# Attention in steps of two duos with its multiplications on GpSimd, and another order around the gather, in a one-core attention and expert kernel

## The reference

```python
scores = scale * q @ k.T                      # per batch and head
keep = (key < n_sink) | (0 <= query - key < window)
a = exp(where(keep, scores, -1e9) - max)
a = a / (sum(a) + 1e-9)
x = (a @ v) as 1536 rows of 512
y = ((x @ w_a) * (x @ w_b)) @ w_out
logits = y @ w_gate                           # 8 experts
# greedy by descending logit: each token to one expert, 192 a expert
out[tokens of e] = relu(y[tokens of e] @ w1[e]) @ w2[e]
```

## Time and profile before

| | us |
|---|---|
| median of 3 runs (lowest, highest) | 624.77 (624.16, 624.82) |
| the profiled execution's own time | 624.48 |
| its span in the profile | 622.6 |
| busy PE | 609.3 (98%) |
| busy DVE, ACT, POOL | 438.1, 290.6, 318.4 |
| PE's share of the chain that ended last | 95% |

### The profile page before, as it was taken

How to read it: one execution, slowest core, us unless ns; L and a number is a source line. 1 busy time by engine, 2 the same in 40 slices (tenths; PEclk the granted TensorE clock), 3 DMA queues, 4 the chain that set the end, 5 groups by cost and what they waited for, 6 DMA issues and landing times.

```text
span 622.6 us, 13278 instructions
## 1 busy us (share of the span) xinstructions
PE 609.3 (98%) x4704; PEld 504.7 (81%) x4704; DVE 438.1 (70%) x1428; ACT 290.6 (47%) x692; POOL 318.4 (51%) x230
## 2 busy tenths in 40 slices
PE   8999999999999999999999999999899999999995
PEld 6666668999899899989977887777677888888894
DVE  6888883333246619999898998888946667766670
ACT  6889883333333332332332224243526756567540
POOL 7566563455455546554456551000094876667741
PEclk9999999999999999999999999999989999999998
DMA  8374231333554364454214151413459578876500
GB/s 277 110 290 147 80 95 55 109 109 102 172 168 122 117 206 133 134 189 120 68 36 153 52 187 37 152 52 114 175 202 386 184 221 294 296 242 238 189 26 25
DMA packets 76096, 94.35 MB, mean 152 GB/s; under 512 B 4448, under 2 KB 53888, under 8 KB 75392
## 3 DMA queue, kind: packets, MB, share of 16 engines
q1 hardware_dynamic: 73696, 86.82, 42.5%
q0 software_dynamic: 2048, 6.29, 3.1%
q10 hardware_dynamic: 288, 0.41, 0.2%
HBM read 87.16 MB, written 6.34 MB: 150 GB/s over the span
## 4 chain that ended last, share of the span: by engine, by line
PE 95%; DVE 2%; POOL 1%; issue 1%; ACT 0%; POOLq 0%; DVEq 0%
PE bank L1392 15%; PE bank L1269 14%; PE bank L1271 13%; PE bank L1270 13%; PE bank L1492 8%; PE bank L1515 5%; PE bank L1256 4%; PE bank L1196 4%; PE bank L1216 4%; PE bank L1494 4%; PE bank L1282 2%; PE bank L1434 2%; PE bank L1343 1%; PE bank L1172 1%; PE bank L1261 1%; PE bank L1474 1%
## 5 line engine op out<-in xcount | busy, mean ns | idle before, releaser
L537 POOL TENSOR_TENSOR wl_ab<-raw_ab,wh_ab 128x1024 fp32r<-128x1024 f32 x46 | 110.1, 2393 | 107.7 <-ACT wh_ab L650 107.7
L1269 PE MATMUL bank<-xh,wh_ab 128*128 128x384 f32 x384 | 131.9, 343 | 0.0
L1271 PE MATMUL bank<-xh,wl_ab 128*128 128x384 f32 x384 | 128.7, 335 | 0.0
L1270 PE MATMUL bank<-xl,wh_ab 128*128 128x384 f32 x384 | 128.6, 335 | 0.0
L607 POOL TENSOR_TENSOR w2l<-w_raw,w2h 128x1024 fp32r<-128x1024 f32 x32 | 75.6, 2388 | 41.9 <-DVE w1l L1083 41.7
L664 ACT ACTIVATE hid<-bank 128x384 f32<-128x384 f32 x48 | 23.6, 491 | 141.9 <-PE bank L1271 141.9
L1269 PEld LDWEIGHTS bank<-xh,wh_ab 128*128 128x128 f32 x384 | 72.0, 188 | 8.2 <-issue 6.3
L970 DVE TENSOR_TENSOR hid<-hid,bank 128x384 f32<-128x384 f32 x48 | 26.5, 553 | 73.3 <-ACT hid L664 73.3
L1492 PE MATMUL bank<-xg,w1h 128*128 128x384 f32 x256 | 75.5, 363 | 1.2 <-issue 1.0
L1270 PEld LDWEIGHTS bank<-xl,wh_ab 128*128 128x128 f32 x384 | 72.2, 188 | 0.0
L1271 PEld LDWEIGHTS bank<-xh,wl_ab 128*128 128x128 f32 x384 | 72.1, 188 | 0.0
(11 more groups left out here) (166 smaller groups left out, 1282.7 us busy)
## 6 DMA issues: line engine op xcount, KB each, us to landing
w_sb<-in_moe_w_dram SPq DMA_DIRECT2D x8, 2048.0 KB, 8.6
w_raw<-in_moe_w_dram SPq DMA_DIRECT2D x32, 512.0 KB, 8.4
raw_ab<-in_moe_w_a_dram SPq DMA_DIRECT2D x48, 256.0 KB, 3.1
raw_ab<-in_moe_w_b_dram SPq DMA_DIRECT2D x48, 256.0 KB, 3.5
raw_out<-in_moe_w_out_dram SPq DMA_DIRECT2D x24, 256.0 KB, 2.7
lb<-logit_rows SPq DMA_DIRECT2D x4, 1536.0 KB, 6.3
v_sb<-in_v_dram SPq DMA_DIRECT2D x8, 384.0 KB
woT<-in_moe_w_outT_dram SPq DMA_DIRECT2D x1, 3072.0 KB, 10.9
```

The lines of the kernel that those rows point to most:

```text
L537: pool.tensor_tensor(wl_ab[s % 2][:, :], raw_ab[s % 3][:, :], wh_ab[s % 2][:, :].bitcast(F32), ALU.subtract).then_inc(abl_done, 1)
L1269: pe.matmul(dst, lh, rh, start=first, stop=False)
L1270: pe.matmul(dst, lh, rl, start=False, stop=False)
L1271: return pe.matmul(dst, ll, rh, start=False, stop=last)
```

## The change

- **Steps of two duos.** 24 steps (`QUADS`, here called quads) replace 48. PE makes the scores of four units, the transposes of both duos two quads back, then both sink transposes of that quad (`turn_sinks`), then the values of both duos three quads back.
- **Banks.** `SB_` has four banks instead of three. The bank `TB` is given up for that: the sinks are turned into unused columns of score banks 1 and 3. The first sink transpose waits until the masks of units 0 and 1 of the current quad are done, the second until all four masks of it are done (`s_masked`), and the next scores into these banks wait until the sinks are copied out (`sinkT_out`). `pe_sb`, `pT_sb` and `sinkT_sb` get 8, 4 and 4 buffers.
- **Multiplications.** `probabilities` on DVE goes. POOL multiplies for both heads, with `tensor_tensor` and the reciprocal broadcast along the row, 96 times.
- **DVE** per quad: one pair of reciprocal instructions for four units, masks 0 and 1, two `x_low`, masks 2 and 3, two sink copies.
- **ACT** per quad: two `x_high`, four exponentials, two copies.
- `KEPT_UP` is 8, 6, 6; pieces of the gated weights at every second quad; `w_outT` is issued after the last pair's loads instead of at pair 3.
- **Tail.** 10 transposes of the identity after the last `y_products`; 2 + 3 instead of 2 + 4 wide products; DVE's `low_w1(0, 2)` waits until POOL has issued both gathers of expert 0 (`gather_issued`), and `low_w1(0, 3)` no longer waits for gathered rows; SP's load of w2 of expert 1 waits for expert 0's rows alone and is split: two quarters, then w1, then two quarters; `expert_in(e + 1)` stands after f = 7 instead of after f = 6.

```diff
-    KEPT_UP = [4, 4, 4, 3]
+    KEPT_UP = [8, 6, 6]
...
-        SB_, PT_, OB_, TB = banks[0:3], banks[3:5], banks[5:7], banks[7]
+        SB_, PT_, OB_ = banks[0:4], banks[4:6], banks[6:8]
+        SINKS = [SB_[i][0:2 * n_sink, MID:MID + P] for i in (1, 3)]
...
                     for h in range(2):
                         sp.wait_ge(yg_in[0][h], 16)
-                        sp.wait_ge(yg_in[1][h], 16)
...
-                if p == 3:
+                if p == PAIRS - 1:
                     sp.dma_start(woT[:, :, :], w_outT).then_inc(woT_in, 16)
...
-            load_w2(1)
+            load_w2(1, range(2))
             load_w1(1)
+            load_w2(1, range(2, 4))
...
             for g in range(DUOS):
...
-                pool.tensor_scalar(pn_sb[g % 4][:, 0:w, h], pe_sb[(2 * g + h) % 6][:, 0:w], inv[:, 2 * g + h:2 * g + h + 1],
-                                   None, ALU.mult).then_inc(pn_ready[h], 1)
+                for h in range(2):
+                    u = 2 * g + h
+                    pool.tensor_tensor(pn_sb[g % 4][:, 0:w, h], pe_sb[u % 8][:, 0:w],
+                                       inv[:, u:u + 1].broadcast_to([P, w]), ALU.mult).then_inc(pn_ready[h], 1)
...
             gather(0)
+            pool.memset(ge_rest[:, 0:1], 0.0).then_inc(gather_issued, 1)
             gather(1)
...
+            for q in range(QUADS + 4):
+                if 0 <= q - 1 < QUADS:
+                    reciprocals(q - 1)
+                if q < QUADS:
+                    mask(4 * q)
+                    mask(4 * q + 1)
+                if q >= 4:
+                    x_low(2 * q - 8)
+                    x_low(2 * q - 7)
+                if q < QUADS:
+                    mask(4 * q + 2)
+                    mask(4 * q + 3)
+                if 0 <= q - 2 < QUADS:
+                    sink_copy(q - 2)
...
+            dve.wait_ge(gather_issued, 1)
             low_w1(0, 2)
-            dve.wait_ge(yg_in[0][0], 16)
             low_w1(0, 3)
...
+            def turn_sinks(q):
+
+                if q % QPP == 0:
+                    return
+                pe.wait_ge(sinkT_out, sinks_before(q))
+                for a in range(2):
+                    pe.wait_ge(s_masked, min(4 * (q + 2) + 2 * a + 2, UNITS))
+                    pe.transpose(SINKS[a], pn_sb[(2 * q + a) % 4][:, P:P + n_sink, :].rearrange("p k h -> p (k h)"),
+                                 ident[:, :]).then_inc(sinkT_ready, 1)
...
+            for q in range(QUADS + 3):
+                if q < QUADS:
+                    for u in range(4 * q, 4 * q + 4):
+                        scores(u)
+                if q < len(KEPT_UP):
+                    keep_clock_up(PT_[1], KEPT_UP[q])
+                if 0 <= q - 2 < QUADS:
+                    turn(2 * q - 4)
+                    turn(2 * q - 3)
+                    turn_sinks(q - 2)
+                if 0 <= q - 3 < QUADS:
+                    values(2 * q - 6)
+                    values(2 * q - 5)
+                if q >= QUADS:
+
+                    gated_half((q - QUADS) // 2, (q - QUADS) % 2)
+            gated_half(1, 1)
...
             y_products(Y_PLACES)
+            keep_clock_up(banks[7], 10)
...
-            keep_clock_up_wide(banks[7], 4)
+            keep_clock_up_wide(banks[7], 3)
...
-                    if f == KF - 2 and e + 1 < E:
-                        expert_in(e + 1)
+                if e + 1 < E:
+                    expert_in(e + 1)
```

More of the change, by code:

```diff
@@ L29, in build @@
     DUOS = UNITS // 2
+    QUADS = DUOS // 2
+    QPP = QT // 2
     KD = DM // P
@@ L400, in load_w1, with load_w2 @@
                              ).then_inc(w1_in[e % 2], 16)
-            def load_w2(e):
+            def load_w2(e, js=range(4)):
                 if e == 0:
@@ L415, in load_w2 @@
                         sp.wait_ge(yg_in[0][h], 16)
-                        sp.wait_ge(yg_in[1][h], 16)
                 if e >= 2:
                     sp.wait_ge(rest_ready, e - 1)
-                for j in range(4):
+                for j in js:
                     if e >= 2:
@@ L491, in _ @@
                 pool.memset(v_sink[i][:, :, :], 0.0).then_inc(v_sink_cleared, 1)
-            for i in range(2):
+            for i in range(4):
                 pool.memset(sinkT_sb[i][:, :], 0.0).then_inc(sinkT_cleared, 1)
@@ L670, in _ @@
             act.dma_start(k_sb[0][:, half:QT, :], kT[0, :, half:QT, :]).then_inc(k_in[0], 16)
[L671 to L694, removed]
@@ new lines, in exps, with pT_copy @@
+            def exps(g):
+                _, n, ns = keys(g % QT)
+                w = n * P + ns
+                for u in (2 * g, 2 * g + 1):
+                    act.wait_ge(s_masked, u + 1)
+                    if g >= 4:
+                        act.wait_ge(pn_ready[u % 2], g - 3)
+                    act.activation(pe_sb[u % 8][:, 0:w], s_sb[u % 4][:, 0:w], ACT.Exp, bias=nmx[:, u:u + 1],
+                                   scale=-1.0, accum_out=rowsum[:, u:u + 1]).then_inc(exp_done, 1)
+            def pT_copy(d):
+                w = P * keys(d % QT)[1]
+                act.wait_ge(pT_ready, d + 1)
+                if d >= 4:
+                    act.wait_ge(pv_done, d - 3)
+                act.activation(pT_sb[d % 4][:, :].rearrange("p (h k) -> p h k", h=2)[:, :, 0:w],
+                               PT_[d % 2][:, :].rearrange("p (h k) -> p h k", h=2)[:, :, 0:w],
+                               ACT.Copy).then_inc(pT_out, 1)
@@ L855, in x_low @@
                                   ALU.subtract).then_inc(xl_done, 1)
[L857 to L866, removed]
-                        dve.wait_ge(sinkT_cleared, 2)
-                    dve.tensor_copy(sinkT_sb[d % 2][0:2 * n_sink, :], TB[0:2 * n_sink, 0:P]).then_inc(sinkT_out, 1)
-                if g >= 5:
-                    x_low(g - 5)
-                d = g - 1
-                if 0 <= d < DUOS:
-                    dve.wait_ge(exp_done, 2 * d + 2)
-                    dve.tensor_scalar(rowsum_eps[:, 2 * d:2 * d + 2], rowsum[:, 2 * d:2 * d + 2], 1e-9, None,
-                                      ALU.add).then_inc(eps_done, 1)
-                    dve.wait_ge(eps_done, d + 1)
-                    dve.reciprocal(inv[:, 2 * d:2 * d + 2], rowsum_eps[:, 2 * d:2 * d + 2]).then_inc(inv_ready, 1)
-                    probabilities(d, 1)
@@ L1223, in gate_rows @@
                     pe.wait_ge(wg_in, 16)
[L1224 removed]
+                    pe.wait_ge(xl_done, DUOS)
                 else:
```

97 lines of the change are left out of this document (51 added, 46 removed).

## The result

The changed kernel takes 617.9 us (median of 4 runs, 617.84 to 619.79), the kernel before 624.8 in the same comparison. The ratio is 0.990, 95% interval 0.988 to 0.992. The prediction was 619.3, range 611.5 to 624.0. The profiled execution took 617.87 (span 616.1, against 622.6), so 6.5 us of span went.

| Event | before | after | gained so far |
| --- | --- | --- | --- |
| scores of duo 10 start | 21.30 | 20.81 | 0.5 |
| first gate rows (woT, wg) | 112.39 | 110.11 | 2.3 |
| wide products of the gather start | 450.62 | 448.31 | 2.3 |
| first product of expert 0 | 459.91 | 455.04 | 4.9 |
| rest rows, expert 1 | 491.18 | 486.30 | 4.9 |

What follows compares the result with a forecast made beforehand. In attention PE was taken as the bound, then a ring through PE and DVE; behind the routing, PE's waits and half-clock fillers. Attention -1.4, gather -2.5 and expert 1 -1.3 from 624.48 gave 619.3 us, range 611.5 to 624.

Steps and rivals of the forecast that it cites:

- main case: Whole kernel: attention -1.4, gather -2.5 and expert 1 -1.3 us give 619.3; chance 0.44.
- PE's own work and the added wait: Attention: PE's work 10.06 us a pair; with the second sink transpose waiting for the fourth mask until 2.64, 11.15 against 11.45.
- A: Attention, step of a pair with scores of a first quad: 2.88 us of PE work, 3.3 with the wait for masks.
- B: Attention, step of a pair with eight transposes, sinks and six value groups: 4.36 us with the wait, not 3.76.
- C: Attention, step of a pair with transposes of a first quad and no sinks: 3.42 us.
- The ring as the bound: Attention: scores, masks, sink transpose, values and next scores wait on each other through PE and DVE; 11.15 us a pair.
- no ring: Rival, attention: masks and sinks get out of each other's way, ACT's 10.3 us a pair bounds; 613.9 us, chance 0.22.
- POOL becomes the bound: Rival, attention: at 1.12 us a multiplication POOL needs 13.4 us a pair; 636 us, chance 0.08.
- Fill and drain: Attention's ends: duo 10's scores start at 20.9, 0.4 us earlier; the end takes 0.9 us more.
- Slow fill: Rival, start of attention: PE's clock falls in gaps of quads 2 to 4, some 3 us double; 622.5 us, chance 0.13.
- The gather: Behind the routing: ten transposes keep the clock up, wide products end at 455.0, PE turns rows 2.5 us earlier.
- Expert 1: Start of expert 1: ACT's 1.26 us wait for w1 goes, -1.3; late w2 would return at most the same.

Runs made afterwards that it cites:

- a4: The changed kernel with DVE's two `x_low` ahead of the four masks instead of between the second and the third: 625.7 us, ratio 1.002.
- a3: The changed kernel with the two sink transposes between the values of the two duos instead of ahead of both: 617.2 us, ratio 0.988.
- b4: The changed kernel with POOL's multiplications as tensor_scalar with the column of reciprocals, instead of tensor_tensor with it broadcast: 622.0 us, ratio 0.995.
- b1: The changed kernel without the ten filler transposes ahead of the gather's index products: 619.0 us, ratio 0.990.
- c1: The changed kernel without POOL's small memset and DVE's wait for it, so DVE makes w1's last two low parts at once: 621.0 us, ratio 0.994.
- b3: The changed kernel with all four quarters of expert 1's w2 asked for ahead of its w1: 617.0 us, ratio 0.987.
- b2: The changed kernel with the next expert's rows turned after f = 6 again, as in the kernel before: 620.5 us, ratio 0.993.
- a1: The changed kernel with all edits around the gather and the experts undone, only attention changed: 621.7 us, ratio 0.994 to the kernel before.

## Why the prediction was right

The main case came in, with 617.9 for 619.3. By its steps:

- *PE's own work and the added wait.* Predicted A 3.3, B 4.36, C 3.42 and 0.07 more: 11.15 a pair. Measured A 3.15 or 3.46, B 4.31, C 3.42: 11.03 a pair ((86.98 - 20.81) / 6, with a like step at 86.98). The added wait stands where it was put (2.64). The mis-sized term is the saving a pair, 0.42 instead of 0.30: over 6.33 pairs 2.7 instead of 1.9. Step A without ACT's piece of the gated weights ahead of `xh` is 3.15, less than the 3.3 assumed for all.
- *The ring as the bound.* Half right. a4 shows that the masks bound the steps with sinks. But a3 took PE's wait for them away and gained 1.3 us by the last scores and 0.8 in all, not the 5.4 that the rival "no ring" adds to the forecast: right behind the ring stands PE's own order with two more changes of kind. ACT was at 0.93 in attention, so its 10.3 a pair is near but not reached.
- *POOL.* Predicted 0.74 of at most 1.12, measured 0.62. The Trainium skill ("GPSIMD Engine Reference", section on engine selection) puts two-input work on GpSimd at about half of VectorE's speed and one-input work at roughly line-rate; for this pair of forms the traces say the opposite, 0.62 for two tensors against 0.97 in b4. The rival "POOL becomes the bound" was a real one: b4 has it, at 0.97 a multiplication, just above the 0.93 from which the prediction let it decide.
- *Fill and drain.* Duo 10 at 20.81 for 20.9. The drain is the rest of attention's 2.3: 0.5 + 2.7 - 2.3 = 0.9, as predicted. Read directly, from the end of the last step with scores (90.4) to the fourth gated half (103.78), it is 13.4 against 12.26, so 1.1 more, and 0.3 of that is the wait for ACT at 90.75, which was in no term. Slow fill did not happen: PE waited 0.73 for ACT at 14.34, and the granted clock was 1.00 from 5 to 21 us.
- *The gather.* Predicted 2.5, measured 2.6. b1 shows that the ten transposes hold the clock and c1 that the gate on DVE keeps the issue short; without either one expert 0 starts 1.3 to 1.5 later. The Trainium skill ("TensorE: Matmul & The Clock Gate", Part 4: PE-mode transpose) says that transposes do not count as activity the same way; here the granted clock behind them was 1.00 with them and 0.50 without, so that rule doesn't hold at this place.
- *Expert 1.* Wrong, predicted -1.3, measured +0.2. The prediction took w2's second half to land before ACT splits it. Its third quarter landed 2.08 late, which was named as the case that gives at most the 1.3 back. It gave back more: against the steady step, 19.17 and before 19.44, the stall grew from 1.38 to 1.83. b3 puts the quarters in front again and gains 0.9.
- *`expert_in` behind f = 7.* Wrong, predicted 0, measured 0.26 for each expert, 1.7 by b2. The prediction had counted products and not changes of kind, though it had priced such a change at 0.15 to 0.20 from the earlier trace rows. The transposes now stand where the kind changes anyway; in the trace 0.17 of the 0.26 stands at these changes, and the rest is open.

So the sum was right within 1.4 us partly by luck: two errors in the experts (+1.5 and -1.8) cancelled. 0.9 of what is left is attention's.

## What to carry to other kernels

Where a change shortens the way to a wait for a load, look up which load is next in that queue: here the tail's gain made w2 late, and undoing part of it (b1) cost only 0.7 of 1.5. Count changes of product kind on PE wherever a block of transposes is moved, not the products alone. And a recorded wait is not the gain of removing it, since what stands behind it may be nearly as late: in a3 the wait for the masks went (2.5 us of PE's products, 6.0 of its weight loads, between 25 and 90 us), and 1.3 us came of it by the last scores, 0.8 by the end.

## What the runs showed of the hardware

- On POOL, 128x260 float32 multiplied by a column of reciprocals took 0.62 us as two tensors with one broadcast and 0.97 (b4) to 1.12 with the column as operand. A small DVE instruction, on `rowsum` (128x4), took 0.17 where POOL was idle beside it and 0.62 beside a two-tensor instruction of POOL (changed kernel, 38.30 to 38.92; POOL's from 38.16 to 38.89). In b4, where POOL is nearly always busy, it took 0.17 to 1.74, on the mean 0.57 between 30 and 60 us. The 0.62 and the 1.74 ended within 0.03 of an end on POOL.
- An indirect gather's issue on POOL took 0.91 to 1.19 us alone and 1.53 (a1) to 3.12 beside DVE's low parts of w1. In c1 it is its own time and the 2.09 that it shares with them (448.43 to 450.52); the third one of the changed kernel lay wholly beside them (451.12 to 453.01) and took only 1.89, so this is no rule yet.
- Of DVE's w1 parts of expert 1, the one that started beside POOL's two-tensor `w2l` took 2.37, the other three 1.21 (b3).
